# Reordering the 512 columns that TensorE streams in each product, pair by pair

## The reference

```python
# x, f_logit: (2, 6080, 256); w_in: (256, 2048); w_out: (2048, 256)
f = lower_bound + (1 - lower_bound) * sigmoid(f_logit)
for t in range(S):
    h = f[:, t] * h + (1 - f[:, t]) * x[:, t]
    y[:, t] = h
x = y.reshape(B * S, D)                       # 12160 tokens of 256
h = x @ w_in
g = where(h > 0, h, exp(minimum(h, 0)) - 1)   # ELU
out = g @ w_out
```

## Time and profile before

| | |
|---|---|
| device time, median of 2 runs | 989.82 us (989.73 to 989.9) |
| span of the profiled execution | 987.9 us |
| TensorE (PE) busy | 983.2 us, 100% of the span, 4362 matmuls |
| TensorE weight loads (PEld) | 817.7 us, 83% |
| ScalarE (ACT) | 791.6 us, 80% |
| VectorE (DVE) | 726.4 us, 74% |
| GpSimd (POOL) | 633.2 us, 64% |

### The profile page before, as it was taken

How to read it: one execution, slowest core, us unless ns; L and a number is a source line. 1 busy time by engine, 2 the same in 40 slices (tenths; PEclk the granted TensorE clock), 3 DMA queues, 4 the chain that set the end, 5 groups by cost and what they waited for, 6 DMA issues and landing times.

```text
span 987.9 us, 15016 instructions
## 1 busy us (share of the span) xinstructions
PE 983.2 (100%) x4362; PEld 817.7 (83%) x4362; DVE 726.4 (74%) x916; ACT 791.6 (80%) x1424; POOL 633.2 (64%) x477
## 2 busy tenths in 40 slices
PE   9999999999999999999999999999999999999998
PEld 6998888888888888888888888888888888888887
DVE  6987876976886796697688679678768867956444
ACT  7988878878888887877887887888788788787775
POOL 2588796576567558557656756856765765675444
PEclk9999999999999999999999999999999999999999
DMA  7212012002102201200210210120021021001001
GB/s 265 66 33 91 0 35 63 33 1 76 54 1 60 69 1 42 64 21 10 65 53 0 64 63 0 51 66 10 25 61 42 0 74 53 0 0 45 1 1 43
DMA packets 23078, 42.02 MB, mean 43 GB/s; under 512 B 2560, under 2 KB 4096, under 8 KB 23040
## 3 DMA queue, kind: packets, MB, share of 16 engines
q1 hardware_dynamic: 22752, 41.10, 12.9%
q10 hardware_dynamic: 288, 0.46, 0.1%
HBM read 29.10 MB, written 12.45 MB: 42 GB/s over the span
## 4 chain that ended last, share of the span: by engine, by line
PE 100%; DVE 0%; POOL 0%; issue 0%; POOLq 0%
PE acc L886 17%; PE acc L888 17%; PE acc L887 17%; PE h L859 14%; PE h L855 14%; PE h L857 14%; PE h L992 1%; PE h L993 1%; PE h L991 1%; PE h L999 1%; PE h L958 0%; PE h L968 0%; PE acc L991 0%; PE acc L992 0%; PE acc L993 0%; PE acc L958 0%
## 5 line engine op out<-in xcount | busy, mean ns | idle before, releaser
L327 POOL TENSOR_TENSOR g_lo<-e,g_hi 128x512 fp32r<-128x512 f32 (+1 forms) x384 | 519.4, 1363 | 348.6 <-ACT g_hi L471 347.7
L457 ACT ACTIVATE e<-h 128x512 f32<-128x512 f32 (+1 forms) x379 | 225.6, 595 | 151.7 <-PE h L859 129.2
L710 DVE SCALAR_TENSOR_TENSOR e<-e,h 128x512 f32<-128x512 f32 (+1 forms) x379 | 256.3, 676 | 70.7 <-ACT e L463 70.4
L887 PE MATMUL acc<-g_lo,w_out_hi 128*128 128x512 f32 (+1 forms) x768 | 297.2, 387 | 0.0
L886 PE MATMUL acc<-g_hi,w_out_hi 128*128 128x512 f32 (+1 forms) x768 | 297.2, 387 | 0.0
L888 PE MATMUL acc<-g_hi,w_out_lo 128*128 128x512 f32 (+1 forms) x768 | 297.2, 387 | 0.0
L463 ACT ACTIVATE e<-e 128x512 f32<-128x512 f32 (+1 forms) x384 | 241.5, 629 | 9.6 <-issue 1.2
L471 ACT CAST g_hi<-e 128x512 fp32r<-128x512 f32 (+1 forms) x384 | 232.4, 605 | 16.9 <-DVE e L710 16.9
L859 PE MATMUL h<-a_hi,w_in_lo 128*128 128x512 f32 x616 | 239.7, 389 | 0.0
L855 PE MATMUL h<-a_hi,w_in_hi 128*128 128x512 f32 x616 | 239.7, 389 | 0.0
L857 PE MATMUL h<-a_lo,w_in_hi 128*128 128x512 f32 x616 | 239.6, 389 | 0.0
(11 more groups left out here) (77 smaller groups left out, 563.0 us busy)
## 6 DMA issues: line engine op xcount, KB each, us to landing
opening<-forget_logit SPq DMA_DIRECT2D x44, 256.0 KB, 2.6
x<-value SPq DMA_DIRECT2D x44, 256.0 KB, 2.7
out<-out_sb SPq DMA_DIRECT2D x44, 256.0 KB, 2.0
w_in_raw<-w_in SPq DMA_DIRECT2D x8, 256.0 KB, 6.1
w_out_raw<-w_out SPq DMA_DIRECT2D x8, 256.0 KB, 6.8
out<-out_sb SPq DMA_DIRECT2D x4, 224.0 KB, 1.9
x<-value SPq DMA_DIRECT2D x3, 224.0 KB, 6.6
opening<-forget_logit SPq DMA_DIRECT2D x2, 224.0 KB, 6.6
```

Of the source, the lines that this page charges most:

```text
L327: nc.gpsimd.tensor_tensor(g_lo[:, t % RING, 0:w], e[:, t % TILES, 0:w], g_hi[:, t % RING, 0:w].bitcast(F32), ALU.subtract).then_inc(g_lo_r ...
L457: nc.scalar.activation(e[:, i, 0:w], bank_of(j, t)[:, 0:w], ACT.Relu, scale=-1.0).then_inc(r_ready, 1)
L710: nc.vector.scalar_tensor_tensor(e[:, t % TILES, 0:w], e[:, t % TILES, 0:w], -1.0, bank_of(j, t)[:, 0:w], ALU.add, ALU.max).then_inc(g_rea ...
L887: nc.tensor.matmul(bank, hi, g_lo[:, t % RING, 0:w], start=False, stop=False)
```

## The change

A table gives each of the eight pairs of units an order in which its matmuls go through the 512 columns. The same order is applied to the moving operand and to the result, so column c of the result is still made from column c of the operand. It is applied in `product` and, for blocks 1 to 11, in `second`; the matmuls of block 0 keep their order.

- pair 0: (1, 512), unchanged
- pairs 1 to 4: runs of 4 columns (16 bytes); the runs are visited in 2, 4, 16 or 64 turns, so that one run and the next lie 8, 16, 64 or 256 columns apart
- pair 5: runs of 32 columns, in two turns (64 columns apart)
- pair 6: runs of 128 columns, in two turns (256 columns apart)
- pair 7: all 512 columns backwards, one at a time

The number of matmuls, their weights, their waits and the rest of the program stay.

```diff
+ORDER = ((1, 512), (2, 4), (4, 4), (16, 4), (64, 4), (2, 32), (2, 128), None)
...
+def in_order(columns, q):
+    if ORDER[q] is None:
+        return columns[:, ::-1]
+    turns, run = ORDER[q]
+    if turns == 1:
+        return columns
+    return columns.rearrange("p (b a c) -> p a b c", a=turns, c=run)
...
-                nc.tensor.matmul(bank[:, 0:w], hi, a_h[:, 0:w], start=start, stop=False,
-                                 skip_group_check=True)
-                nc.tensor.matmul(bank[:, 0:w], hi, a_l[:, 0:w], start=False, stop=False,
-                                 skip_group_check=True)
-                return nc.tensor.matmul(bank[:, 0:w], lo, a_h[:, 0:w], start=False, stop=True,
-                                        skip_group_check=True)
+                into = in_order(bank[:, 0:w], q)
+                a_h, a_l = in_order(a_h[:, 0:w], q), in_order(a_l[:, 0:w], q)
+                nc.tensor.matmul(into, hi, a_h, start=start, stop=False, skip_group_check=True)
+                nc.tensor.matmul(into, hi, a_l, start=False, stop=False, skip_group_check=True)
+                return nc.tensor.matmul(into, lo, a_h, start=False, stop=True, skip_group_check=True)
...
-                bank = acc[:, b, half, 0:w]
-                nc.tensor.matmul(bank, hi, g_hi[:, t % RING, 0:w], start=opens, stop=False)
-                nc.tensor.matmul(bank, hi, g_lo[:, t % RING, 0:w], start=False, stop=False)
-                done = nc.tensor.matmul(bank, lo, g_hi[:, t % RING, 0:w], start=False, stop=closes)
+                bank, g_h, g_l = acc[:, b, half, 0:w], g_hi[:, t % RING, 0:w], g_lo[:, t % RING, 0:w]
+                if not first:
+                    bank, g_h, g_l = in_order(bank, q), in_order(g_h, q), in_order(g_l, q)
+                nc.tensor.matmul(bank, hi, g_h, start=opens, stop=False)
+                nc.tensor.matmul(bank, hi, g_l, start=False, stop=False)
+                done = nc.tensor.matmul(bank, lo, g_h, start=False, stop=closes)
```

## The result

The changed kernel takes 1040.4 us (median of two runs, 1040.38 to 1040.42) against 989.82 us. The ratio is 1.0511, with a 95% interval of 1.0466 to 1.0556. The forecast was 989.8 us.

What follows compares the result with a forecast made beforehand. TensorE's matmul stream was taken to bound the kernel, with no cover. Count, issuing, signals and stream order all added nothing: 987.9 + 0 us, plus 1.9 us from span to median, gave 989.8 us; range 985 to 1110 us.

Steps and rivals of the forecast that it cites:

- What bounds the kernel: TensorE, busy the whole span: number of matmuls times their distance, 0.2267 us each at 512 columns, with no cover.
- Steps 1 to 3: 3465 matmuls reordered, 785.5 of 987.9 us; longer operand descriptions cost nothing to issue; semaphore signals do not move.
- Step 4: The 512-column stream from SBUF to PSUM: no price for any pair's order, since 16-byte pieces stay whole; less confident for backwards.
- The nearest row, a VectorE sum: VectorE's sum over w_in_raw: four runs of 128 columns in 678 ns, unbroken row 689; long runs cost that engine nothing.
- The reading of the 13.4 ns: At every 512-column matmul, the remainder over 213.3 ns looks like a fixed cost of starting one.
- The gain that I gave 2 in 100: Rival: some order of the reordered streams is quicker, at most 46 us off, 944 us; chance 0.02.
- The upper end: Slow warm-up matmuls, 0.426 us apart, taken as half rate: 213 ns on each of 3465 matmuls, 738 us more, 1728 us.
- Backwards: Rival in pair 7: 495 matmuls at half rate, 213 ns more each, 105.6 us, 1095 us in all; chance 0.2.
- A cycle per run: Rival at run ends: 0.417 ns a run, 53.3 ns in pairs 1 to 4, 110 us together, 1100 us; chance 0.13.
- Halved streams: Rival: any gap halves the stream; pairs 1 to 4 add 422 us, 1412 us, up to 1728 us; chance 0.1.
- The sign that was named for this case: Differing distances among pairs 1 to 4 would mean run spacing, not number, costs, and step 4 is wrong.
- The range: For 8 in 10, 985 to 1110 us: takes in rivals at 1095 and 1100, leaves out halved streams and the quick one.

Runs made afterwards that it cites:

- e10: Changed kernel with all eight pairs in the order of pair 3, runs of four columns at jumps of 256 bytes: 1193.1 us.
- e8: Changed kernel with all operands read rising; only second products write PSUM in harder orders (runs of two columns, (16, 4), backwards): 989.6 us.
- e2: Changed kernel with another table for pairs 1 to 7: (8, 4), (32, 4), (2, 2), (16, 2), (2, 8), (2, 16), (4, 8): 1261.3 us.
- e4: Changed kernel with all eight pairs in runs of four columns in four turns (jumps of 64 bytes): 976.6 us, ratio 0.9867 to the kernel before.
- e11: Kernel before, every pair rising, with the moving operands 128 bytes further in SBUF and the weights in place: 1013.0 us, ratio 1.0234.
- e6: Changed kernel with other orders of four-column pieces: falling pieces, falling blocks of 2, 4 and 8, four turns falling, falling columns inside pieces: 1023.3 us.
- e9: Changed kernel with another table for pairs 1 to 7: runs of 32, 64 and 128 bytes at jumps of 256 to 1024 bytes: 1034.1 us.
- e14: Kernel before, every pair rising, with the moving operands 256 bytes further in SBUF and the weights in place: 990.0 us.
- e18: e4 with the moving operands 192 bytes further in SBUF: 989.2 us, ratio 0.9995 to the kernel before.
- e17: e4 with the moving operands 64 bytes further in SBUF and the weights in place: 975.7 us, ratio 0.9857 to the kernel before.
- e15: Kernel before, every pair rising, with the moving operands 64 bytes further in SBUF and the weights in place: 998.0 us.
- e12: e4 with four turns only where first products read and second products write, the other sides rising: 997.0 us, ratio 1.0074 to the kernel before.

## Why the prediction was wrong, point by point

- **What bounds the kernel** was right: TensorE's stream alone, with no cover. Every added ns reached the end: 50.7 us by the distances, 50.6 us by the times, and e10 was forecast to 1 us by counting.
- **Steps 1 to 3** (3465 reordered matmuls, nothing for issuing, nothing for the signals) held. No idle time appeared before a matmul, and e8, where one of the two operands of the second products has a description as long as in the change, runs in the old time.
- **Step 4 failed, and within it one sentence**: that a memory which delivers 16 bytes at a time "serves the same pieces, each once, only in another order". The 16-byte pieces are real for the reading (e2), but which piece follows which has a price of its own: from -3.4 ns for (4, 4) alone in the kernel to +51.4 ns for (16, 4). I had weighed the number of pieces and not their sequence. The nearest row, a VectorE sum, spoke of another engine and of four runs; it could not carry pairs 1 to 4, as the prediction itself says before it takes nothing for them.
- **The reading of the 13.4 ns** as a fixed cost of starting a matmul was wrong too. The remainder hangs on order and place: it becomes 10 ns in e4 and 19 in e11, with the same number of starts. The trace of the kernel before already spoke against a fixed cost. Its last warm-up matmuls, bf16 and as wide, start 216 ns apart, 2.7 ns over the 213.3. They differ in type, place and weight load, so they don't say what the other 10.7 ns are, but the start of a bf16 matmul costs no more than 2.7. And the distances behind the earlier trace rows are not alike: they go through 203, 199, 207 and 202 ns. "It stands at every matmul alike" was taken for a sign of a fixed cost; it was a stream in lockstep. The gain that I gave 2 in 100 exists, at 13 us instead of the bound of 46, though in an order that the change used in one pair of eight. Two of those warm-up matmuls, from the first's start to the second's end, where one lasts 0.38 us:

```profile
6.78 0.59 PE L999 MATMUL h<-e 128*128 128x512 bf16 x2
```

- **The upper end** came from the earlier trace rows, which can't bear it. The same warm-up instruction, on the same operands, starts 427 ns apart up to 6.4 us and 216 ns apart from 6.8 us on, close to 512 columns at 1.2 and at 2.4 GHz, so the slow ones fit the lower clock level and tell nothing of a slow way of reading, though the granted clock reads 1.00 over both stretches. The 213 ns taken from them as the price of half the rate came near the 225 ns of e2 by luck.
- **The rivals.** Backwards has a price, 7 ns and not 213: 3.5 us in all. A cycle per run is near for (16, 4) (51 ns against 53 forecast) and far off for (2, 4) and (4, 4), which have the same 128 runs and cost 5 and -1 ns in the changed kernel. Halved streams do exist, but among the orders tried only for runs of 8 bytes, which the change has not. The sign that was named for this case, "if distances differ among pairs 1 to 4, it is the spacing of the runs and not their number that costs", is what came, though e6 and e9 show that the spacing alone doesn't set the price either.
- **The range** took in 1095 and 1100 us, and so 1040 us lies inside it, but by luck: each rival had one price for all orders, and the sum stood at nothing or at 105 us and more. A price for each spacing between those ends is what the case asked for.

**What stays open.** Why just these sequences are dear. A return to the same place modulo 256 bytes fits (16, 4), (32, 4) and (64, 4) to within 5 ns at a cycle a jump (273, 267 and 253 ns against 278, 268 and 252), and e14 finds the same modulus, which would suit parts of SBUF that repeat every 256 bytes and are slow to be asked twice running. That is a guess, and it doesn't explain the blocks of four falling pieces (267 ns), nor 231 against 248 ns for runs of 32 bytes at 512 and 256 bytes. How the small prices come about between the moving stream and the weights (e11 to e18) is not shown either; weights loaded in another order were not tried.

## What to carry to other kernels

When TensorE streams without a gap, its distance from start to start is a measure of how the moving operand is fetched; compare it with columns over clock before calling the rest a fixed cost. Read fp32 operands in whole pieces of 16 bytes, keep runs of 16 bytes at jumps of 128 bytes or more, the dear ones here, out of the reading side (246 to 278 ns), and move any reordering that is needed to the PSUM side, where it was free. Where a kernel's time is all TensorE, try the place of the moving operands against the weights in steps of 64 bytes, and runs of four in four turns for all matmuls: here the two were worth from -1.4% (e17) to +2.3% (e11).

## What the runs showed of the hardware

- The moving operand in fp32r behaves as if fetched in 16-byte pieces, at about 1.77 ns each for 512 columns in rising order; half-used pieces cost the same (451 ns against 226.7, e2).
- A bf16 matmul of 512 columns starts 216 ns after the one before, an fp32r one 226.7 ns (both in the kernel before).
- Writing to PSUM in gaps, in runs of 8 bytes, or backwards: no cost (226.7 ns in all eight pairs of e8).
- The order of the pieces read is worth 223.3 to 278.1 ns for the same 512 columns (e4, e10).
- A shift of the moving operands by 128 bytes against the weights: +5.7 ns a matmul, 23 us; by 64 bytes +2.2 ns; by 256 bytes nothing (e11, e15, e14).
- A matmul's read order is felt by those after it, up to the seventh: the rising stream takes 226.7 ns among its own and 230.5 between four-turn ones (e12).
- A weight load of 128 columns lasts 188 ns beside rising streams and 193 beside (16, 4) (e10).
